# A new start for a fused attention and two-layer expert kernel: first scores kept in PSUM, some operands left unsplit in fp32

## What is computed

```python
kv_pool = kv.reshape(B, H//4, 4, W//4, 4, C).mean(axis=(2, 4))   # 768 keys
k = v = kv_pool.reshape(B, -1, C) @ w_sr                         # C = 128
s = (q @ k.T) / sqrt(C);  s = s - s.max(-1)                      # 12288 queries
a = exp(s);  a /= a.sum(-1) + 1e-9
x = a @ v
h = x @ moe_w_in                                                 # d_ff = 2048
g = where(h >= 1, h, where(h <= -1, 0, (h + 1)**2 / 4))
y = g @ moe_w_out
h = y @ moe2_w_in;  out = (h * sigmoid(1.702 * h)) @ moe2_w_out
```

## Time and profile before

| | us |
|---|---|
| median of 3 runs | 1334.9 |
| lowest, highest | 1333.6, 1335.53 |
| profiled execution, its own time | 1335.95 |
| its span, first to last instruction | 1334.1 |
| TensorE busy | 1272.2 (95%) |
| GpSimd busy | 1176.6 (88%) |
| ScalarE, VectorE busy | 1022.0 (77%), 1019.6 (76%) |

### The profile page before, as it was taken

How to read it: one execution, slowest core, us unless ns; L and a number is a source line. 1 busy time by engine, 2 the same in 40 slices (tenths; PEclk the granted TensorE clock), 3 DMA queues, 4 the chain that set the end, 5 groups by cost and what they waited for, 6 DMA issues and landing times.

```text
span 1334.1 us, 17190 instructions
## 1 busy us (share of the span) xinstructions
PE 1272.2 (95%) x5496; PEld 1037.7 (78%) x5496; DVE 1019.6 (76%) x1165; ACT 1022.0 (77%) x1083; POOL 1176.6 (88%) x481
## 2 busy tenths in 40 slices
PE   4567999999999999999999999999999999999988
PEld 3455888888888888888888888888888888878866
DVE  6788787797797787887877877977878878756433
ACT  3666778887878878788788878788787887886756
POOL 1668999999999999999999999999999999998760
PEclk9778999999999999999999999999999999999999
DMA  9100010010000000100000100000000000000000
GB/s 340 40 16 16 9 33 17 16 32 16 16 24 24 16 16 16 32 16 16 32 16 16 32 16 16 27 20 16 16 16 32 16 17 24 9 17 16 0 9 16
DMA packets 18605, 36.19 MB, mean 27 GB/s; under 512 B 3344, under 2 KB 3472, under 8 KB 18320
## 3 DMA queue, kind: packets, MB, share of 16 engines
q1 hardware_dynamic: 18576, 35.83, 8.3%
HBM read 29.43 MB, written 6.39 MB: 27 GB/s over the span
## 4 chain that ended last, share of the span: by engine, by line
PE 80%; POOL 8%; issue 6%; DVE 2%; DMA 2%; ACT 1%; SPq 0%; POOLq 0%; DVEq 0%; ACTq 0%
PE ps_ring L353 15%; PE ps_ring L354 15%; PE ps_ring L355 15%; PE ps_y L353 12%; PE ps_y L355 11%; PE ps_y L354 11%; POOL g_lo L306 3%; POOL g_lo L313 2%; POOL pt_lo L320 2%; DMA kv_sb<-in_kv_t 1%; DVE s_sb L707 1%; DMA key_max<-max_row 1%; DMA max_row<-max_turned 0%; SPq L231 0%; DVE g L758 0%
## 5 line engine op out<-in xcount | busy, mean ns | idle before, releaser
L313 POOL TENSOR_TENSOR g_lo<-g,g_hi 128x1024 fp32r<-128x1024 f32 x192 | 523.5, 2727 | 81.6 <-DVE g L758 74.7
L306 POOL TENSOR_TENSOR g_lo<-g,g_hi 128x1024 fp32r<-128x1024 f32 x181 | 436.4, 2411 | 4.6 <-ACT g_hi L577 4.6
L751 DVE SCALAR_TENSOR_TENSOR g_hi<-g,ps_ring 128x1024 fp32r<-128x1024 f32 x192 | 233.6, 1216 | 152.9 <-ACT g L591 148.8
L575 ACT ACTIVATE g<-ps_ring 128x1024 f32<-128x1024 f32 x192 | 197.2, 1027 | 179.3 <-PE ps_ring L355 179.1
L353 PE MATMUL ps_y<-g_hi,w_hi 128*128 128x512 f32 x768 | 304.7, 397 | 24.4 <-POOL g_lo L313 20.2
L355 PE MATMUL ps_y<-g_hi,w_lo 128*128 128x512 f32 x768 | 301.0, 392 | 0.0
L354 PE MATMUL ps_y<-g_lo,w_hi 128*128 128x512 f32 x768 | 301.0, 392 | 0.0
L758 DVE SCALAR_TENSOR_TENSOR g<-g,ps_ring 128x1024 f32<-128x1024 f32 x192 | 232.9, 1213 | 0.0
L584 ACT ACTIVATE g<-ps_ring 128x1024 f32<-128x1024 f32 x192 | 198.0, 1031 | 20.3 <-POOL g_lo L313 14.2
L591 ACT ACTIVATE g<-g 128x1024 f32<-128x1024 f32 x192 | 204.2, 1064 | 5.4
L577 ACT ACTIVATE g_hi<-ps_ring 128x1024 fp32r<-128x1024 f32 x192 | 195.9, 1020 | 5.1 <-PE ps_y L355 5.1
(11 more groups left out here) (69 smaller groups left out, 1752.7 us busy)
## 6 DMA issues: line engine op xcount, KB each, us to landing
kv_sb<-in_kv_t SPq DMA_DIRECT2D x12, 512.0 KB, 8.4
q_sb<-in_q_t SPq DMA_DIRECT2D x24, 256.0 KB, 3.7
key_max<-max_row SPq DMA_DIRECT2D x24, 256.0 KB, 3.4
inv_sum<-inv_row SPq DMA_DIRECT2D x24, 256.0 KB, 3.2
out_t<-y_sb SPq DMA_DIRECT2D x24, 256.0 KB, 3.4
w_raw<-in_moe_w_in SPq DMA_DIRECT2D x2, 1024.0 KB, 16.8
max_row<-max_turned SPq DMA_DIRECT2D x24, 2.0 KB, 1.3
inv_row<-inv_turned SPq DMA_DIRECT2D x24, 2.0 KB, 1.3
```

What stands on the lines that cost most here:

```text
L306: nc.gpsimd.tensor_tensor(g2_lo[:, slot, :], g2[:, slot, :], g2_hi[:, slot, :].bitcast(F32), ALU.subtract).then_inc(g2_lo_done, 1)
L313: nc.gpsimd.tensor_tensor(g1_lo[:, slot, :], g1[:, slot, :], g1_hi[:, slot, :].bitcast(F32), ALU.subtract).then_inc(g1_lo_done, 1)
L575: nc.scalar.activation(g2[:, slot, :], ps_h2(k), ACT.Gelu_apprx_sigmoid).then_inc(g2_done, 1)
L751: nc.vector.scalar_tensor_tensor(out=g1_hi[:, uu % 2, :], in0=g1[:, uu % 2, :], scalar=1.0, in1=ps_h1(k), op0=ALU.min, op1=ALU.max).then_i ...
```

## The change

**First tile.** Its scores stay in PSUM (all three ring slots). The maxima are not sent through DRAM: VectorE multiplies an identity pattern by their upper and lower parts (`spread_first_maximum`), and TensorE multiplies these by a matrix of -1 and adds into the scores (`subtract_maximum`, 12 passes). ScalarE exponentiates from PSUM. VectorE adds the six chunks of exponentials (`add_first_keys`), TensorE multiplies by ones (`spread_sums`, unsplit fp32), and VectorE takes the reciprocal of all 128x512 sums (`normalise_first`).

**Keys.** The first projection takes 512 keys instead of 384, and the first four score chunks follow it before the second.

**Values of tiles 0, 1 and 2** are unsplit: `exp` output times `v_sb`, one fp32 matmul a chunk in place of three passes; `probs_upper` and `probs_lower` fall away for them. **Layer 1's output** for tiles 0 and 1 (16 units) is unsplit: `g1` times `w_raw`; `unit_upper` and `g1_lo` fall away.

**Order.** Tile 2's and tile 3's scores follow each other after step 7 of iteration 2; iteration 3 is written out. POOL now writes the upper halves of three of the four weights as well (`w_upper`), and the lower halves of `w_out1`, which overwrite `w_raw`, at the start and in step 4 of iteration 4.

```diff
@@ pool @@
+            def w_upper(m):
+                pool.wait_ge(w_loaded[m], 16)
+                    nc.gpsimd.tensor_copy(w_hi[:, cols], w_raw[:, cols]).then_inc(w_hi_done[m], 1)
             def iteration(it, half):
+                if is_number(it, PLAIN // U + 2):
+                    pool.wait_ge(g1_used, PLAIN - U // 2)
+                    w_lower(1, 0)
...
+                    if k == 4 and is_number(it, PLAIN // U + 2):
+                        pool.wait_ge(g1_used, PLAIN)
+                        w_lower(1, 1)
...
+            pool.wait_ge(x_lo_done, 1)
+            w_upper(2)
+            q_lower(2, q2_lo[:, :], q2_sb[:, :], q2_hi[:, :])
+            w_lower(2, 0)
+            w_lower(2, 1)
+            pool.wait_ge(shifted, PAIRS)
+            w_upper(3)
+            q_lower(3, q_lo[:, :], q_sb[:, 1, :], q_hi[:, :])
+            w_lower(3, 0)
+            w_lower(3, 1)
+            pool.wait_ge(v_hi_done, 1)
+            lower(v_lo[:, :, :], v_sb[:, :, :], v_hi[:, :, :]).then_inc(v_lo_done, 1)
+            w_upper(1)
@@ tensor @@
+            def subtract_maximum():
+                pe.wait_ge(ones_ready, 2)
+                for part, spread in enumerate((spread_hi, spread_lo)):
+                    pe.wait_ge(max_masked, part + 1)
+                    for c in range(KC):
+                        last = nc.tensor.matmul(ps_s(0, c), minus_ones[:, :], spread[:, :], start=False,
+                                                stop=(part == 1), skip_group_check=True)
+            def spread_sums():
+                pe.wait_ge(keys_added, 5)
+                nc.tensor.matmul(ps_y2[:, :], ones[:, :], key_sums[:, 4, :], start=True,
+                                 stop=True).then_inc(sums_spread, 1)
+                if whole(t):
+                    nc.tensor.matmul(ps_o(t), v_sb[:, c, :], s_keys(t, t % 2, c), start=(c == 0),
+                                     stop=(c == KC - 1)).then_inc(pv_done, 1)
+            def layer_out_plain(dst, m, u, r):
+                    last = nc.tensor.matmul(dst[:, :], w_raw[:, f], r[:, d * T:(d + 1) * T],
+                                            start=(u == 0 and d == 0), stop=(u == U - 1 and d == 1))
...
+            subtract_maximum()
+            for c in range(4):
+                value_chunk(0, c)
+            spread_sums()
+            for c in range(4, KC):
+                value_chunk(0, c)
             for k in range(U):
                 step(2, 0, k)
+            values_then_scores(1, 2, 3)
+            for k in range(U):
+                step(3, 1, k)
@@ scalar @@
+            step(2, 0, 2)
+            step(2, 0, 3)
+            step(2, 0, 4)
+            exponential(1, 1, 0)
+            step(2, 0, 5)
+            exponential(1, 1, 1)
+            exponential(1, 1, 2)
+            step(2, 0, 6)
+            step(2, 0, 7)
+            evacuate(2, 0)
+            evacuate(3, 1)
+            x_upper(1, 1)
@@ vector @@
+            def normalise_first():
+                nc.vector.tensor_scalar(inv_sum[:, :], ps_y2[:, :], 1e-9, None, ALU.add).then_inc(eps_added, 1)
+                nc.vector.reciprocal(inv_sum[:, :], inv_sum[:, :]).then_inc(inverted, 1)
+                nc.vector.tensor_tensor(x_hi[:, 0, :], ps_o(0), inv_sum[:, :], ALU.mult).then_inc(x_hi_done, 1)
+                nc.vector.tensor_tensor(x_sb[:, :], ps_o(0), inv_sum[:, :], ALU.mult).then_inc(x_done, 1)
+                x_lower(0, 0)
...
+            unit_full(2, 4)
+            shift(1, 1, 1)
+            shift(1, 1, 2)
+            unit_full(2, 5)
             for p in range(PAIRS):
+                add_keys(1, 1, p)
+            unit_full(2, 6)
             invert(1)
+            unit_full(2, 7)
```

More of the change, by code:

```diff
@@ L127, in encoder_kernel @@
         q_loaded = sem("q_loaded")
+        q2_loaded = sem("q2_loaded")
         w_scaled = sem("w_scaled")
@@ L195, in iterations @@
         def iterations(eng, body):
-            for it in range(RAMP, 2 * LOOP_FIRST):
+            for it in range(4, 2 * LOOP_FIRST):
                 body(it, it % 2)
@@ L329, in iteration @@
                     if k == 3 and is_tile(it + 1):
[L330 to L341, removed]
-            q_lower(3, 1)
-            for p in range(PAIRS):
-                probs_lower(1, 1, p)
-            for k in range(5, U):
-                step(2, k)
-            w_lower(3)
+                        q_lower(it + 1, q_lo[:, :], q_sb[:, 1 - half, :], q_hi[:, :])
+                    if k == 4 and is_number(it, PLAIN // U + 2):
+                        pool.wait_ge(g1_used, PLAIN)
+                        w_lower(1, 1)
+            q_lower(0, q_lo[:, :], q_sb[:, 0, :], q_hi[:, :])
+            pool.wait_ge(k_copied, 1)
+            pool.wait_ge(k_hi_done, 1)
+            lower(k_lo[:, 0:FIRST_KEYS], k_sb[:, :], k_hi[:, 0:FIRST_KEYS]).then_inc(k_lo_first, 1)
+            q_lower(1, q1_lo[:, :], q_sb[:, 1, :], q1_hi[:, :])
+            w_lower(0, 0)
+            w_lower(0, 1)
+            pool.wait_ge(x_lo_done, 1)
[12 more added lines that the diff above has]
+            for k in range(U):
+                step(3, k)
+                if k == 3:
+                    q_lower(4, q_lo[:, :], q_sb[:, 0, :], q_hi[:, :])
             iterations(pool, iteration)
@@ new lines, in score_chunk @@
+                if in_ramp(t):
+                    if t == 3 or t > 0 and c >= 2:
+                        pe.wait_ge(s_early, (t - 1) * KC + c - 1)
+                elif c >= 2:
+                    pe.wait_ge(s_evac, (t - RAMP) * KC + c - 1)
+                keys = slice(c * P, (c + 1) * P)
+                upper, lower = q_hi, q_lo
+                if is_number(t, 1):
+                    upper, lower = q1_hi, q1_lo
+                if is_number(t, 2):
+                    upper, lower = q2_hi, q2_lo
@@ new lines, in score_chunk @@
+                three_passes(ps_s(t, c), k_hi[:, keys], k_lo[:, keys], upper[:, :],
+                             lower[:, :]).then_inc(scores_ready, 1)
+            def subtract_maximum():
[5 more added lines that the diff above has]
+                                                stop=(part == 1), skip_group_check=True)
+                        if part == 1 and c % 2 == 1:
+                            last.then_inc(max_subtracted, 1)
@@ L747, in unit_upper @@
                 exists, tt, uu, n = unit(it, k, FIRST1)
-                if exists:
+                if exists and not plain(n):
                     dve.wait_ge(square_done, n + 1)
```

528 lines of the change are left out of this document (331 added, 197 removed).

## The result

The changed kernel takes 1322.5 us (median of 4 runs, 1321.79 to 1324.28) against 1335.22 for the one before (four runs now, three in the table above): ratio 0.9908, 95% interval 0.9893 to 0.9924. It is 12.7 us faster; the forecast was 21.3, and its range of 1306 to 1321 ends 1.5 us short of the result. The profiled execution is the shortest of the four (1321.79), with a span of 1320.0.

What follows compares the result with a forecast made beforehand. TensorE, busy 95% of the span, was taken as the bound; a ramp 24.4 us shorter, less 1.4 and 1.7 given back in iteration 4, made 21.3 us, from 1334.9 to 1313.6 us, range 1306 to 1321.

Steps and rivals of the forecast that it cites:

- The even middle and its pace: Iterations after the ramp: TensorE takes a fixed number of passes, 51.9 us an iteration, the same after the change.
- the path to mark 1: From the start to the first pass of layer 1, forecast at 45.9 us against 58.55, 12.7 sooner.
- the loop to mark 2: Units 0 to 3, then values and scores, up to step 0 of iteration 3: 79.3 us against 100.24.
- VectorE's backlog: Iteration 3: 10 us of maxima, subtractions and folds make `y1_lo` ready at 96.3 where TensorE could take it at 93.
- the sign: Whole kernel: the change makes it faster, chance 0.97.
- The masks: First tile: masks put behind GpSimd's `w_lower(0)`, ending at 32.3 us instead of 30.7, costing only a few tenths.
- the clock's fall behind mark 1: After TensorE's 4.6 us idle before layer 1's first pass it runs at half clock; 1.7 us added.
- To mark 3: From step 0 of iteration 3 to `x_sb` of iteration 4, forecast at 125.1 us against 149.49, 24.4 sooner.
- Given back in iteration 4: Iteration 4 loses 1.4 us to four unsplit units and 1.7 to GpSimd's lateness from the moved `w_lower(1)` halves.
- from span to median: Forecast span 1312.8 us became median 1313.6, taking the profiled time as 1.85 above its span and 1.05 above the median.
- GpSimd becomes the bound: Rival: GpSimd's lag after the moved weight halves repeats, about 8 us in place of 1.7, so 1320 us; chance 0.10.
- a falling clock: Rival: iteration 2's 20 us of passes run at half clock and handoffs are longer, 10 us lost, 1323; chance 0.10.

Runs made afterwards that it cites:

- warm: Changed kernel plus 18 unused passes before layer 1's first pass and 14 before tile 1's first output product; 1319.83 us.
- late_lo: Changed kernel with GpSimd's second lower half of `w_out1` moved from step 4 of iteration 4 to the head of iteration 5; 1319.18 us.
- dve_lo: Changed kernel with the second lower half of `w_out1` computed by VectorE at step 7 of iteration 4 instead of GpSimd; 1317.99 us.
- plain20: Changed kernel with 20 instead of 16 units of layer 1 unsplit and the first `w_out1` lower half moved to iteration 5's head; 1319.74 us.
- best: plain12 with iteration 3 reordered: `y1_lo` before two subtractions and the folds, tile 2's exponentials behind step 4; 1319.23 us.
- plain12: Changed kernel with 12 instead of 16 units of layer 1 unsplit and the second `w_out1` lower half written in iteration 3; 1321.75 us.

## Why the prediction missed

**Met.** The even middle and its pace; the path to mark 1, 0.55 us late, where the reciprocal took 3.35 against 3.3 and the unsplit fp32 matmuls their 0.86 (0.43 a half from start to start); the loop to mark 2, where the outputs of units 0 to 3 start at 52.54, 55.72, 58.83 and 61.94 and the values of tile 1 follow at 63.66, within 0.5 us of the ends stepped through (the last 63.2); VectorE's backlog, with `y1_lo` at 97.15 against 96.3; the sign. The masks did stand behind GpSimd's weight part, already with the cast of 32x16 (1.47 us at 29.75). That mark 2 is right to 0.1 us is in part luck: I priced the clock's fall behind mark 1 at 1.7 us, and the runs without it are only 0.8 to 0.95 us faster to mark 2; the 0.8 too much hid mark 1's 0.55 and 0.3 of the rest of the loop.

The row of the reciprocal reads 3.35 us for 512 columns, 6.5 ns a column with the fixed part. The Trainium skill, "VectorE: DVE Perf Modes", section "First, the fixed hardware budget", gives a repeat count of 8; the estimate of 4.3 us that I made of it is not borne out: the measurement decides.

**Step "To mark 3", 3.3 us short.** 0.5 of it is mark 1. I named the wait for `y1_lo` but put no low clock behind it, though I had put one behind the wait at mark 1 on the evidence of the ramp before. warm takes away both falls and 2.55 us, of which 1.66 behind mark 2; that is the second one, which I had put at nothing. The remaining 1.2 is `y1_lo` 0.85 later than stepped, and 0.3 that I can't place.

**Step "Given back in iteration 4", 3.9 us short.** GpSimd made TensorE lose 4.0 us instead of 1.7: 3.52 at 169.94 and 0.44 at 160.84 (0.89 us for two passes, 160.29 to 161.18). Two of its lower parts ahead of 169.94 took 1 us more than the others, beside VectorE's subtractions; that this made the difference to the forecast is an argument from the rows, which no run tests. And behind this wait too the clock fell, 1.6 us where TensorE has no slack, which I had put at nothing. 2.3 and 1.6 are the 3.9. late_lo, dve_lo and plain20 show the cause of the wait, GpSimd's load with the moved weight half: each takes the long wait away and 2.3 to 2.7 us of the time from mark 1 to iteration 6.

**The rest** of the 8.9 us between 1313.6 and 1322.5, 1.7, is how I went from span to median: I took the profiled execution as 1.05 above the median, as before, and after it was 0.7 below.

**The rivals.** "GpSimd becomes the bound" and "a falling clock", 0.10 each and priced at 6 and 10 us, neither came as written: GpSimd's lateness ends with iteration 4 (51.78 us for the one after), and iteration 2 ran at low clock only at its start. But a part of each mechanism came, 2.3 us more lateness than forecast and 3.3 of low clock at two waits where the forecast had none. I had let either happen alone and gave the range no room for the two together.

## What to carry to other kernels

A wait of TensorE that a forecast leaves in the ramp costs itself and then, often, work at low clock: 0.8 to 1.7 us behind most waits of these runs, up to 2.9 (best). In a stretch that TensorE bounds nothing gives either back: price both, at every such wait and not only at the first. The length of the wait alone doesn't tell whether the clock falls. From 20 us on, in the fourteen profiles of this case, it fell behind every wait of 2.92 us and more, behind none of 1.7 and less, and in between it went either way. Work moved off a short start onto an engine that is 95% busy in the loop behind it comes back as a wait there; moving it again only moves the wait, and what helps is taking load off that engine (unsplit operands for four more units) for as long as the debt lasts. Where totals differ by no more than runs do, compare stretches between fixed instructions, and look at the granted clock in each: with the same clock they repeat to 0.1 us.

## What the runs showed that I had not expected

A wait of 2.89 us left TensorE's clock at full (plain12), one of 2.92 at the same place of the work let it fall (best), and that one fall made 2.9 us of difference, more than the 1.5 to 1.7 of the others, since nearly all of the 7 us behind it ran at low clock. Shorter waits do it too: 2.06 us before 1179.79 in the changed kernel, with the clock at 0.91 from 1170 to 1190. A GpSimd instruction with a single SBUF input is much cheaper than with two: a 128x1024 rounding copy takes 1.05 us (six of them, 6.1 us in all), a subtraction 2.4. And a VectorE cast of no more than 32x16 took 1.47 us beside a GpSimd subtraction.
